# A Silu activation on ScalarE in place of Sigmoid on ScalarE and a product on VectorE, in the second of two gated Strassen layers

## The reference

```python
def _moe_ref(x, w_gate, w_val, w_out):
    gate = 1.0 / (1.0 + np.exp(-(x @ w_gate)))
    val = x @ w_val
    return (gate * val @ w_out).astype(np.float32)

def _moe2_ref(x, w_gate, w_val, w_out):
    g = x @ w_gate
    silu = g * (1.0 / (1.0 + np.exp(-g)))
    val = x @ w_val
    return (silu * val @ w_out).astype(np.float32)
```

## Time and profile before

| what | value |
|---|---|
| time, median of 3 runs | 1857.26 us (1855.51 to 1858.43) |
| time of the profiled execution | 1854.75 us |
| its span in the profile | 1853.0 us |
| TensorE matmul busy | 1767.3 us, 95% |
| TensorE weight load busy | 1718.7 us, 93% |
| VectorE busy | 1275.2 us, 69% |
| ScalarE busy | 895.1 us, 48% |
| GpSimd busy | 363.7 us, 20% |
| mean granted TensorE clock | 0.991 |

### The profile page before, as it was taken

One profiled execution on the slowest core, in us unless ns is written; L12 is line 12 of the kernel. 1 busy time (PEld: TensorE's weight loads), 2 busy tenths in 40 slices (PEclk: granted clock), 3 DMA queues, 4 the chain that ended last, 5 costly groups with the idle time before them and its releaser, 6 DMA issues.

```text
span 1853.0 us, 30995 instructions
## 1 busy us (share of the span) xinstructions
PE 1767.3 (95%) x11184; PEld 1718.7 (93%) x11184; DVE 1275.2 (69%) x2041; ACT 895.1 (48%) x1676; POOL 363.7 (20%) x326
## 2 busy tenths in 40 slices
PE   6799999998999999999999999998999999999997
PEld 5698898998999999999998899998999998999997
DVE  3566766776766668666679888887766678666665
ACT  3455655654444445444445555554444454444444
POOL 5522222103211124111143000013111124111111
PEclk9999999999999999999999999999999999999999
DMA  9777687556655566666555455565656565455452
GB/s 202 207 236 222 181 270 233 194 196 212 238 188 188 195 230 220 211 205 211 202 196 186 180 191 190 190 211 175 216 188 205 204 229 196 146 188 183 181 181 79
DMA packets 201561, 368.52 MB, mean 199 GB/s; under 512 B 49856, under 2 KB 161472, under 8 KB 201408
## 3 DMA queue, kind: packets, MB, share of 16 engines
q1 hardware_dynamic: 201408, 366.53, 59.2%
HBM read 234.36 MB, written 130.55 MB: 197 GB/s over the span
## 4 chain that ended last, share of the span: by engine, by line
PE 75%; DVE 8%; issue 7%; DMA 5%; ACT 2%; POOL 2%; SPq 2%; DVEq 0%; POOLq 0%; ACTq 0%
PE ps L685 70%; DVE arena L1100 2%; DVE arena L1113 1%; PE ps L593 1%; DVE hop L1061 1%; PE ps L578 1%; DMA wops<-in_q_dram 1%; PE ps L626 1%; PE ps L583 1%; DMA wops<-in_v_dram 1%; DVE xo L983 1%; DVE arena L1128 1%; DMA wops<-in_moe_w_gate_dram 1%; DVE wa L978 1%; PE ps L603 1%
## 5 line engine op out<-in xcount | busy, mean ns | idle before, releaser
L685 PE MATMUL ps<-xo,wa 128*128 128x384 f32 x6048 | 1090.2, 338 | 17.9 <-ACT arena L843 5.9
L685 PEld LDWEIGHTS ps<-xo,wa 128*128 128x128 f32 x6048 | 1053.3, 189 | 26.7 <-ACT arena L843 8.0
L1100 DVE TENSOR_TENSOR arena<-ps,arena 128x384 f32<-128x384 f32 x648 | 351.3, 553 | 359.2 <-PE ps L685 282.0
L843 ACT ACTIVATE arena<-ps 128x384 f32<-128x384 f32 x648 | 317.3, 490 | 559.7 <-PE ps L685 558.9
L685 PE MATMUL ps<-hop,wb 128*128 128x384 f32 x3024 | 551.2, 339 | 24.3 <-DVE arena L1128 5.9
L685 PEld LDWEIGHTS ps<-hop,wb 128*128 128x128 f32 x3024 | 527.5, 190 | 38.6 <-DVE arena L1128 9.1
L1061 DVE TENSOR_TENSOR hop<-arena,hop 128x384 fp32r<-128x384 f32 (+1 forms) x396 | 286.8, 747 | 33.8 <-ACT hop L825 26.8
L1282 POOL TENSOR_TENSOR arena<-arena 128x384 f32<-128x384 f32 x144 | 145.6, 1033 | 777.7 <-DVE arena L1100 777.5
L825 ACT ACTIVATE hop<-arena 128x384 fp32r<-128x384 f32 (+1 forms) x396 | 233.6, 608 | 68.2 <-DVE arena L1128 40.5
L864 ACT ACTIVATE arena<-arena 128x384 f32<-128x384 f32 x216 | 112.5, 521 | 94.4 <-DVE arena L1100 94.2
L1128 DVE TENSOR_TENSOR arena<-arena 128x384 f32<-128x384 f32 x216 | 129.8, 602 | 13.5
(11 more groups left out here) (61 smaller groups left out, 877.4 us busy)
## 6 DMA issues: line engine op xcount, KB each, us to landing
xo<-x_operands SPq DMA_DIRECT2D x168, 768.0 KB, 6.3
x_operands<-xo SPq DMA_DIRECT2D x84, 768.0 KB, 4.5
x<-arena SPq DMA_DIRECT2D x120, 384.0 KB, 3.6
arena<-x SPq DMA_DIRECT2D x96, 384.0 KB, 4.3
xraw<-x SPq DMA_DIRECT2D x22, 768.0 KB, 6.3
out_dram<-wops SPq DMA_DIRECT2D x48, 192.0 KB, 2.1
wops<-in_k_dram SPq DMA_DIRECT2D x22, 288.0 KB, 4.1
wops<-in_v_dram SPq DMA_DIRECT2D x22, 288.0 KB, 5.2
```

What stands on the lines that cost most here:

```text
L685: mm = pe.matmul(dst, lhsT, rhs, start=(pr in (1, 5, 2) and c == 0 and i == 0), stop=(c == 1 and i == 2), skip_group_check=(pr in (6, 7, 4 ...
L843: nc.scalar.activation(dst, X(side), ACT.Copy).then_inc(copied, 1)
L1100: nc.vector.tensor_tensor(dst, acc, buf, ALU.add).then_inc(summed, 1)
```

## The change

In layer 2, ScalarE applies `Silu` where it applied `Sigmoid`, and in the place where layer 1 writes it: over the gate's sum, or to `c21_buf`. The VectorE product `silu` (line 1113) and its semaphore are gone, and everyone who waited for it waits for `sig_done`. Both layers now share one path (`gated`, line 851 in the changed kernel). The buffer `sg` is still there, since the late attention uses it.

```diff
@@ bank_free, TensorE @@
-                            elif place(pq)[0] == 0:
+                            else:
                                 pe.wait_ge(sig_done, n_hid(pq, pw, 21))
-                            else:
-                                pe.wait_ge(silu_done, n_silu(pq, pw, 21))
@@ ScalarE @@
-                    def sigmoid(c):
+                    def gated(c):
...
-                        if l == 0:
-                            dst = c21_buf if c == 21 else src
-                            if c == 21 and g > 0 and pw < 2:
-                                act.wait_ge(h_done, n_hid(pq, pw, 21))
-                            elif c == 21 and g > 2:
-                                act.wait_ge(h_done, n_hid(pq, 1, 21))
-                        else:
-                            dst = sg[:, {11: 0, 22: 1, 21: 0, 12: 1}[c]]
-                            if c in (21, 12):
-                                act.wait_ge(silu_done, n_silu(qq, w, {21: 11, 12: 22}[c]))
-                            elif n_silu(qq, w, c) > 4:
-                                act.wait_ge(silu_done, n_silu(qq, w, 11) - 1)
-                        nc.scalar.activation(dst, src, ACT.Sigmoid).then_inc(sig_done, 1)
+                        dst = c21_buf if c == 21 else src
+                        if c == 21 and g > 0 and pw < 2:
+                            act.wait_ge(h_done, n_hid(pq, pw, 21))
+                        elif c == 21 and g > 2:
+                            act.wait_ge(h_done, n_hid(pq, 1, 21))
+                        nc.scalar.activation(dst, src, (ACT.Sigmoid, ACT.Silu)[l]).then_inc(sig_done, 1)
@@ VectorE @@
-                    def silu(c):
-                        src = {11: p_buf[:, 0], 22: u3_buf[:, 0], 21: X(0), 12: u2_buf[:, 0]}[c]
-                        dst = c21_buf if c == 21 else src
-                        dve.wait_ge(sig_done, n_hid(qq, w, c))
-                        nc.vector.tensor_tensor(dst, src, sg[:, {11: 0, 22: 1, 21: 0, 12: 1}[c]], ALU.mult
-                                                ).then_inc(silu_done, 1)
-
                     def hidden(c):
...
-                        if l == 0:
-                            dve.wait_ge(sig_done, n_hid(qq, w, c))
-                        else:
-                            dve.wait_ge(silu_done, n_silu(qq, w, c))
+                        dve.wait_ge(sig_done, n_hid(qq, w, c))
```

More of the change, by code:

```diff
@@ L231, in strassen_mlps @@
         sig_done = sem("sig_done")
-        silu_done = sem("silu_done")
         h_done = sem("h_done")
@@ L256, in n_hid @@
             return 8 * qq + 4 * w + HID[c] + 1
-        def n_silu(qq, w, c):
-            return n_hid(qq - QN // 2, w, c)
         def n_hop(qq, pr, c):
@@ L931, in _ @@
                             if w < 2:
-                                sigmoid(11)
+                                gated(11)
                             if is_late(u + 1):
@@ L941, in _ @@
                             if w < 2:
-                                sigmoid(22)
+                                gated(22)
                             if is_late(u + 1):
@@ L950, in _ @@
                             if w < 2:
-                                sigmoid(21)
+                                gated(21)
                                 hop_split(1, w)
@@ L955, in _ @@
                         if s == 11 and w < 2:
-                            sigmoid(12)
+                            gated(12)
                         if s == 12 and w == 2 and p == 0:
@@ L1167, in _ @@
                             total(22, 1)
-                        if l == 1:
-                            silu(11)
                         hidden(11)
@@ L1174, in _ @@
                             total(22, 1)
-                        if l == 1:
-                            silu(22)
                         hidden(22)
@@ L1181, in _ @@
                             split_x(nxt, 2)
-                        if l == 1:
-                            silu(21)
                         total(12, 0)
@@ L1187, in _ @@
                         total(12, 1)
-                        if l == 1:
-                            silu(12)
                         hidden(12)
```

## The result

The changed kernel takes 1836.0 us (median of 5, 1835.4 to 1837.7) against 1857.3, a ratio of 0.989 (95% interval 0.9875 to 0.9904). A second set of six executions, beside others of the kernel before, gave 1838.6 against 1855.4, 0.9911 (0.9897 to 0.9926). So the gain is 21.3 us in one set and 16.7 in the other; the forecast was 21.6, and 1835.7 us.

A forecast was written before the change was run, and what follows sets the result against it. TensorE bounds nine floor blocks of layer 2 (gain 0), VectorE block 18. The other blocks give 3.0 + 6.2 + 6.8 + 5.6 = 21.6 us, from 1857.26 to 1835.7 us; forecast's own range 1832 to 1841, overall 1830 to 1845.

The forecast's parts named there:

- The twin: Layer 1 blocks do layer 2's work without the product; the difference prices blocks 19 to 22, 23, 24, 29 and 30.
- Borders 23 and 29: First blocks of two pairs at borders between passes in layer 2: gains of 2.4 and 1.0 us from layer 1 counterparts.
- Block 18: First block of layer 2, bound by VectorE, no counterpart: gain between 0.75 and 7.5 us, taken as 5.6.
- The 0.9 us for the clock: Block 18, window 2: 66 matmuls take 13.22 us after a gap, 12.29 in block 19 after none.
- VectorE's freed time: Layer 2: eight products fewer a block, 0.59 us each, free 4.7 us of VectorE; nothing gained in nine floor blocks.
- The bank and the buffers: Quarter 21: ScalarE's read frees the bank and its sigmoid needs no `sg` buffer; inside the other terms, no own size.
- The table load: One load of 1.28 us ahead of the first Silu, covered by ScalarE's rest: 0, or 1.28 us without the cover.
- The clock: Granted clock falls after TensorE gaps in blocks 18, 23, 29 and 30; mean clock would become 1.00 there.
- Only the waits that are named come back: Rival: TensorE regains only its 10.0 us of waits for line 1113 in layer 2; 1847.3 us, chance 0.14.
- Block 18 and more: Rival: block 18 gives 7.5 us and the borders some more; gain 24 to 27 us, 1830 to 1833, chance 0.10.
- the rival on the slower side: Silu is dear on ScalarE's path in 36 gated windows: slower from 1.7 us a Silu, 1872 at 2.1; chance 0.04.

The follow-up runs named there:

- runs with spare products: Changed kernel plus idle-result VectorE products at the old products' places: all 144, 1862.7 us; 72 of them, 1848.2; with a PSUM input in blocks 18 to 30, 1856.0.

## Why the prediction was right, and where not

**The twin.** In the first profile blocks 19 to 22, 24 and 30 came out within 0.03 us of their counterparts in layer 1, 12.5 us of the gain in all (in the second, block 30 was 0.2 off). This is the step that carried the forecast. Borders 23 and 29 came within 0.8 and 1.1 us, in opposite directions. For 23 that is the spread from one execution to the next; block 29 was below its twin in all five profiles without the products, so there the twin priced it too low. In block 30, 1.6 of the 5.8 us were the clock behind its gap, which may fall or not; the profile that the forecast was read from had it.

**Luck.** That the first median lies within 0.3 us of the forecast is luck. The blocks make 18.1 us of the 21.6, and the second set gained 16.7. The range of 1832 to 1841 was put together right but for its upper end: 4.85 us less in block 18 and 1.5 us of spread give 1842.

**Block 18.** This term was mis-sized: 5.6 us expected, 1.9 and 2.1 measured. I took it near its upper end "because VectorE hardly rests here". VectorE did get the time free: it was busy 50.46 us before and 44.41 after, 6.1 us less, more than the 4.7 that I counted. The block did not follow. By the traces, ScalarE's queue now waits longer in its place, 2.94 us for x (1.15 before) and 1.93 for the weights (0.80 before): both were already almost as late. With the products back the block took 53.5 to 55.9 us in four profiles, VectorE busy 49.4 to 50.3 of them. The forecast had looked at one engine's busy time and not at which transfer lands next. The 0.9 us for the clock did not show either: the block is at 1.00 now, but from the first matmul of window 2 to the block's end are 17.7 us, and 17.6 before, since TensorE now stops for 1.45 us three matmuls into it (1027.77). What the block gained, 2.0 us, is all ahead of window 2.

**VectorE's freed time.** I had 0.59 us a product and a busy time down by 79 us; it is 63 us, 0.44 a product. VectorE in order of time, window 0 of block 18 after:

```profile
1007.53 0.55 DVE L1087 TENSOR_TENSOR arena<-ps,arena 128x384 f32<-128x384 f32 x1
1008.18 0.56 DVE L1105 TENSOR_TENSOR arena<-arena 128x384 f32<-128x384 f32 x1
```

Two `hidden` products behind each other (from 1005.05) take 1.02 us in one piece, and one right behind the sum that it needs starts 0.65 us after it (1007.53 to 1008.18), where instructions that don't depend on each other follow in 0.47. It seems that the product had partly stood in such a gap, which is still there. This did no harm to the forecast, since only block 18 was computed from it.

**The bank and the buffers.** I had named both as part of the gain and put no number on them. In the runs with spare products no block shows a saving by them.

**The table load.** Costed at 0. The run without the load took 1835.6 us and is not told from 1836.0, and up to the wait for x the load cost block 18 0.03 us. Two loads in a window were not hidden at the floor, 44.92 us against 43.68.

**The clock.** The falls in blocks 18, 29 and 30 are gone as forecast. That of block 23 is not, though the gap before it is shorter than the 3.49 us before. TensorE in block 23 after, and in block 5 of layer 1 before:

```profile
1259.27 1.32 PE L679 MATMUL ps<-hop,wb 128*128 128x384 f32 x6 [1.99 <-DVE arena L1105]
...
439.62 1.31 PE L685 MATMUL ps<-hop,wb 128*128 128x384 f32 x6 [1.99 <-DVE arena L1128]
```

The clock of block 23 is 0.97 after a gap of 1.99 us, and that of block 5 was 1.00 after a gap of the same length (50.49 us). A gap of this length can bring a fall or not.

**The rivals.** "Only the waits that are named come back", 10.0 us, would have been 1847: the blocks gained 18.1, and the second set 16.7. The waits' total counts only the stops that the product itself ended, not those that it made longer for others. "Block 18 and more" fails with block 18. Silu is not dear, so the rival on the slower side never came near the 1.7 us at which it decides.

## What to carry to other kernels

If a kernel does the same work twice, once with the operation and once without, the difference of two blocks of its own trace is the price to start from: here it had the knock-on effects in it, and six blocks came out as it said. Take it at the same granted clock on both sides, or name the clock's part. Where there is no such twin and one engine is busy all the time, the freed time is an upper bound: look for the next transfer or queue that is nearly as late, and take a value nearer to the neighbours. And the fused activation cost nothing here, where its tables stay loaded: count the loads in the order of instructions, one a stage and not one a window.

## What was not expected of the hardware

- GpSimd and VectorE slow each other down when VectorE reads two tensors from the shared storage: a product of 0.55 us took up to 1.11, a GpSimd difference of 0.7 to 0.9 took 2.5; with one input in PSUM the product stayed at 0.54 to 0.56.
- The same wait of 1.8 us cost 1.6 us more in the execution in which the granted clock fell behind it (49.19 against 47.58 us in block 30). With gaps of 1.8 to 2.0 us it went either way, and this makes part of the spread of the totals.
- Two table loads with a tiny activation between them take 2.8 us in a row on ScalarE: 1.28 us for each load, 0.20 for the activation, and nothing between them.
